# Expert 0's first slot tile taken from three batches, beside the routing of the last batch

## What is computed

```python
logits = np.einsum('bsd,de->bse', x, w_gate)
local_gate = 1.0 / (1.0 + np.exp(-np.einsum('bsd,de->bse', x, w_local).squeeze(-1)))
for b in range(B):
    prev_e = -1
    for s in range(S):
        fresh_e = int(np.argmax(logits[b, s]))
        e = fresh_e if s == 0 or local_gate[b, s] < 0.5 else (prev_e if prev_e >= 0 else fresh_e)
        prev_e = e
        h = np.maximum(x[b, s] @ w1[e], 0.0)
        out[b, s] = p[e] * (h @ w2[e])      # p is the softmax of logits[b, s]
```

## Time and profile before

| | |
|---|---|
| median of 3 runs | 882.67 us (881.75 to 883.35) |
| profiled execution | 882.88 us |
| its span, first to last instruction | 881.0 us |
| PE busy | 806.8 us, 92% of the span |
| POOL, DVE, ACT busy | 521.6, 447.2, 387.8 us |
| mean DMA rate | 140 GB/s |

### The profile page before, as it was taken

The page is one execution under the profiler, slowest core; times in us unless marked ns, Lnnn a source line. Parts: engine busy times, 40 slices in busy tenths (PEclk is TensorE's granted clock), DMA queues, the critical chain, the costliest instruction groups (busy, mean ns, idle before and its releaser), DMA issues. The chain is left out here.

```text
span 881.0 us, 16450 instructions
## 1 busy us (share of the span) xinstructions
PE 806.8 (92%) x5056; PEld 680.1 (77%) x5057; DVE 447.2 (51%) x1042; ACT 387.8 (44%) x667; POOL 521.6 (59%) x461
## 2 busy tenths in 40 slices
PE   6989999999999525999999999998488999999998
PEld 3768788788887314888888888886377899898998
DVE  5768888888878371222212221222085756645622
ACT  2658787887878331121212212121275534524310
POOL 4547767766778806845898989996265703404100
PEclk9999999999999956999999999999699999999999
DMA  7976787787674336574665655560310110110101
GB/s 184 343 181 172 188 197 181 175 199 192 166 169 120 114 128 215 160 256 167 239 181 187 179 190 166 192 227 36 114 36 19 48 61 25 38 47 1 47 10 54
DMA packets 78758, 123.42 MB, mean 140 GB/s; under 512 B 26176, under 2 KB 39744, under 8 KB 78720
## 3 DMA queue, kind: packets, MB, share of 16 engines
q1 hardware_dynamic: 68912, 100.13, 39.6%
q0 software_dynamic: 3472, 11.28, 4.3%
q10 hardware_dynamic: 6336, 11.54, 4.0%
HBM read 70.55 MB, written 23.86 MB: 107 GB/s over the span
## 5 line engine op out<-in xcount | busy, mean ns | idle before, releaser
L330 POOL TENSOR_SCALAR p_ring<-p_ring,xs_nat 128x576 f32<-128x576 f32 x144 | 105.9, 751 | 82.8 <-DVE xs_nat L437 82.8
L407 DVE TENSOR_REDUCE xs_nat<-psum 128x1 f32<-128x576 f32 x144 | 105.9, 749 | 44.4 <-PE psum L518 35.9
L422 DVE SCALAR_TENSOR_TENSOR p_ring<-psum,xs_nat,e_ring 128x576 f32<-128x576 f32 x144 | 114.5, 811 | 14.7 <-PE psum L564 9.6
L1166 PE MATMUL psum<-w_split,h_hi 128*128 x352 | 116.8, 403 | 3.2 <-DVE h_lo L1230 3.2
L518 PE MATMUL psum<-k_st,q_st 128*128 128x288 f32 x600 | 115.2, 318 | 4.5 <-issue 4.3
L1145 PE MATMUL psum<-w_split,x_hi 128*128 x352 | 117.3, 405 | 1.9 <-DVE x_lo L1225 1.9
L1072 POOL TENSOR_TENSOR w_split<-w_raw,w_split 128x1024 fp32r<-128x1024 f32 x48 | 115.4, 2404 | 4.0
L648 ACT ACTIVATE e_ring<-psum,xs_nat 128x576 f32<-128x576 f32 x144 | 105.7, 750 | 14.9 <-DVE xs_nat L407 14.0
L666 ACT COPY p_t<-psum 128x512 f32<-128x512 f32 x144 | 84.5, 587 | 32.4 <-PE psum L553 29.4
L518 PEld LDWEIGHTS psum<-k_st,q_st 128*128 128x128 f32 x600 | 85.5, 192 | 15.4 <-DVE p_ring L422 10.7
L1352 POOL TENSOR_TENSOR stage<-g,xs_nat 128x512 f32<-128x512 f32 (+1 forms) x20 | 27.3, 1365 | 110.0 <-ACT xs_nat L1558 110.0
(11 more groups left out here) (184 smaller groups left out, 1581.1 us busy)
## 6 DMA issues: line engine op xcount, KB each, us to landing
w_raw<-w_dram SPq DMA_DIRECT2D x48, 512.0 KB, 3.4
k_st<-k_split SPq DMA_DIRECT2D x60, 320.0 KB, 5.4
q_st<-q_split SPq DMA_DIRECT2D x60, 144.0 KB, 2.6
xs_dram<-stage SPq DMA_DIRECT2D x23, 256.0 KB, 2.3
xs_nat<-xs_dram ACTq DMA_DIRECT2D x22, 256.0 KB, 2.8
ys_dram<-y_nat ACTq DMA_DIRECT2D x22, 256.0 KB, 2.2
k_nat<-k_t_dram SPq DMA_DIRECT2D x15, 320.0 KB, 4.2
out_dram<-out_sb SPq DMA_DIRECT2D x32, 144.0 KB, 1.8
```

The source lines that it names most:

```text
L330: pl.tensor_scalar(t, t, rsum[:, col:col + 1], 1.0, ALU.mult, ALU.mult).then_inc(s_norm, 1)
L407: dve.tensor_reduce(negmax[:, u % 3, 0:1], s_bank[u % 3][:, :, 0:HALF], AX.XY, ALU.max, negate=True).then_inc(s_max, 1)
L422: dve.scalar_tensor_tensor(out=p_tile[u].rearrange("p (a b) -> p a b", a=2), in0=s_bank[u % 3][:, :, 0:HALF], scalar=thresh[:, u % 3:u % 3 ...
L1166: mm = pe.matmul(py, a[:, f, :], rhs.rearrange("p o n -> p (o n)"), start=(n == 0), stop=(n == len(terms) - 1))
```

## The change

- The three blocks up to the experts become one, with no barrier in between (`joined`). Everything `route` and `experts` need in SBUF is laid beside or over the attention's buffers (`place`).
- The routing is written anew in two halves, `last=0` for batches 0 to 2 and `last=1` for batch 3. Its pieces are called from the other engines' programs: DVE's `logits_early` and `fresh(0)` stand in pair 14, `rows(0)` in pair 15, and `early` behind the attention; PE's `rows`, `experts`, `ranks` and `first` for batches 0 to 2 stand in pair 15.
- `early` ends in the source rows of expert 0's first tile (`keep["ahead"][:, 0]`). POOL fetches that tile (`x_first`) before batch 3 is routed, and the hops of batch 3's routing stand between the matmuls of `up(0)` and `down(0)`. Tile 1's rows come from `next_tile`, all the others from `sources`.
- Expert 0's eight weight pieces are split one each in pairs 8 to 13 and two in pair 14; before one each in pairs 12 and 13, two in pair 14, three in pair 15 and one in the routing.
- Expert 1's low parts go from POOL to DVE (`low`), behind the routing; ACT's casts (`high`) stand between its work on tile 0. POOL gathers the tiles from the fourth on (23 of them, as before) in one run.
- There is one slot more (26 for 25), one zero-filled piece of 256 KB more, a second constant array of 128 KB (`order_const`), and a first one that is 125 columns wide for 339.

```diff
-SLOTS = (BATCH * SEQ - EXPERTS) // P + EXPERTS
+SLOTS = (BATCH * SEQ + P - EXPERTS) // P + EXPERTS
...
-        pair(ITER - 2, 0, pieces=((1, 0),))
-        pair(ITER - 2, 1, pieces=((1, 1),))
-        pair(ITER - 1, 0, pieces=((0, 2), (1, 3)))
-        pair(ITER - 1, 1, ahead=False, pieces=((0, 4), (1, 5), (1, 6)))
+        for r in range(6):
+            pair(ITER - 4 + r // 2, r % 2, pieces=((1, r),))
+        pair(ITER - 1, 0, pieces=((0, 6), (1, 7)))
+        routing["pool"]["constants"](pl)
+        pair(ITER - 1, 1, ahead=False)
...
+                if isinstance(i, int) and 2 * i + m == PAIRS - 2:
+                    routing["vector"]["logits"](dve)
+                if isinstance(i, int) and 2 * i + m == PAIRS - 1:
+                    routing["vector"]["rows"](dve, 0)
...
+    def early(v):
+        link(v, v.memset(e_row[0:EARLY, SEQ:ST * P], 0.0))
+        follow(v, 0)
+        for a in others:
+            link(v, v.memset(a[:], 1.0))
+            link(v, v.memset(a[:, :, 0:1], 0.0))
+        count(v, 0)
+        places(v, 0)
...
+        lanes(v, 0)
+        v.wait_ge(s_hop, 4)
+        token(v, keep["ahead"][:, 0:1], first_at, 1, "first")
...
+    def lanes(v, last):
+        at = columns(last)
+        for k in range(at.start, at.stop):
+            link(v, v.tensor_scalar(hot_lane[:, k, :], bf["lane"][:], lane[:, k:k + 1], None, ALU.is_equal), f"lane{k}")
...
+        transposes_x(0, x_first, s_first[0])
+        hop["rows"](pe, 1)
+        up(0, halves=range(1), part=range(0, 8))
+        hop["experts"](pe, 1)
+        up(0, halves=range(1), part=range(8, 12), ready=False)
+        hop["ranks"](pe, 1)
+        up(0, halves=range(1, 2), ready=False).then_inc(s_up, 1)
+        transposes_h(0)
+        hop["next"](pe)
+        down(0, part=range(0, 14))
+        hop["sources"](pe)
+        transposes_x(1, xs[:, 1, :], s_first[1])
+        down(0, part=range(14, 24), ready=False).then_inc(s_done, 1)
+        reached(pe, "tables")
+        up(1).then_inc(s_up, 1)
+        transposes_x(2, xs[:, 0, :], s_first[2])
         last = rounds(pe)
-        with pe.Fori(0, last) as j:
+        with pe.Fori(1, last) as j:
...
+        for r in range(3, 7):
+            high(r)
+        x_high(1)
+        high(7)
+        store(0)
+        relu(1)
+        x_high(2)
+        load(3)
...
+        h_low(0)
+        r["all_tiles"](v)
+        r["tables"](v)
+        x_low(1)
+        r["sources"](v)
+        r["weights"](v)
+        for n in range(4):
+            low(n)
+        y_out(0)
+        x_low(2)
+        for n in range(4, PIECES):
+            low(n)
```

More of the change, by code:

```diff
@@ L606, in pair @@
                 scores(n_i, n_m, 1)
+            if isinstance(i, int) and 2 * i + m == PAIRS - 1:
+                pe.wait_ge(s_mask, tile(i, m, 7) + 1)
+                routing["tensor"]["rows"](pe, 0)
             if here:
@@ L616, in pair @@
                 turned(i, m, 5)
+                if isinstance(i, int) and 2 * i + m == PAIRS - 1:
+                    routing["tensor"]["experts"](pe, 0)
                 values(i, m, 0)
@@ L631, in pair @@
                 turned(i, m, 8)
+                if isinstance(i, int) and 2 * i + m == PAIRS - 1:
+                    routing["tensor"]["first"](pe)
         pe.wait_ge(s_zero, 5)
@@ new lines, in route, with sources, weights @@
+    units_row = place("units_row", [1, SLOTS + 1], F32)
+    def sources(v):
+        v.wait_ge(s_hop, 9)
+        token(v, keep["source"][:], source_at, SLOTS, "source")
+    def weights(v):
+        link(v, v.scalar_tensor_tensor(out=tile[:], in0=tile[:], scalar=float(P), in1=lane[:], op0=ALU.mult, op1=ALU.add))
+        link(v, v.tensor_scalar(keep["index"][:].rearrange("p t b -> p b t"), tile[:].rearrange("p (b t) -> p b t", t=ST),
+                                -1.0, None, ALU.add))
+        v.wait_ge(s_exp, 1)
+        link(v, v.tensor_reduce(total[:], less, AX.X, ALU.add))
+        link(v, v.tensor_scalar(total[:], total[:], 1e-9, None, ALU.add))
+        link(v, v.reciprocal(total[:], total[:]))
+        for last in range(2):
+            at = columns(last)
+            link(v, v.tensor_tensor(sel[:, :, at], less[:, at, :].rearrange("p k e -> p e k"), hot[last][:], ALU.mult))
+        link(v, v.tensor_reduce(chosen[:], sel[:].rearrange("p e k -> p k e"), AX.X, ALU.add))
+        link(v, v.tensor_tensor(keep["weight"][:], chosen[:], total[:], ALU.mult), "weights")
@@ new lines, in reached @@
+    def reached(engine, name):
+        engine.wait_ge(step, STEP[name])
+    return {
+        "vector": {"logits": logits_early, "fresh": fresh, "rows": rows, "early": early, "last_logits": last_logits,
+                   "below_top": below_top, "follow": follow, "count": count, "places": places, "lanes": lanes,
+                   "tile_numbers": tile_numbers, "next_tile": next_tile, "next_source": next_source,
+                   "all_tiles": all_tiles, "tables": tables, "sources": sources, "weights": weights},
+        "tensor": {"rows": rows_pe, "experts": experts_pe, "ranks": ranks_pe, "first": first_pe, "next": next_pe,
+                   "sources": sources_pe},
+        "pool": {"constants": constants},
+        "scalar": {"exps": exps},
+        "reached": reached,
+    }
@@ L1722, in build @@
[L1722 to L1731 removed]
+                offset = [behind]
```

711 lines of the change are left out of this document (410 added, 301 removed).

## The result

| | median us | runs | ratio to before, 95% interval |
|---|---|---|---|
| before | 883.01 | 4 (881.75 to 883.74) | |
| after | 873.23 | 4 (872.13 to 875.36) | 0.9894 [0.9869, 0.9918] |
| forecast | 864.0 | range 858.5 to 872 | |

Faster, as forecast, but by 9.8 us instead of 18.8, and 1.2 us outside the range. The profiled execution after took 874.16 us with a span of 872.4. The changed kernel was measured in two more sessions and gave 873.30 and 872.54; the kernel before gave 888.92 and 881.11 beside it (0.9801 [0.9777, 0.9826] and 0.9902 [0.9873, 0.9931]). So the changed kernel repeats within 1 us, while the kernel before moves by several from session to session, and the gain came out at 9.8, 15.6 and 8.6 us.

A forecast was written before the change was run, and what follows sets the result against it. PE bounds attention and experts, with a routing hole near 310 us. Attention would end 2.6 + 1.9 us later, yet `down(1)` 18.8 us earlier (369.51 to 350.7), with nothing lost afterwards: 882.88 - 18.8 = 864.1; range 858.5 to 872.

The forecast's parts named there:

- behind the marker I cost everything at nothing: After the start of `down(1)`, no further loss: PE busy without a gap, weight splits ahead of need; 0 us.
- the marker: Start of `down(1)` on PE, up to which gain was summed; forecast to move from 369.51 to 350.7, 18.8 us less.
- The weight pieces: Attention: five pairs (8 to 12) with a POOL piece slowed by 0.43 each, 1.7 us later (0.4 to 2.6).
- The start: PE's wait for stacked keys near 48 us grows by 0.8 us from 0.28 MB more DMA (0 to 1.0).
- DVE in pairs 14 and 15: Seven more DVE instructions, about 2.7 us, mostly covered by its waits for PE; cost 0.1 us (0 to 1.5).
- The lanes and the order: Attention's end: last values wait for `first` and 15 lanes of 0.25 us; 1.9 us later (1.1 to 3.4).
- From the attention's end to the marker: Chain from 306.1: `up(0)` at 309.3, PE waits 336 to 340.1, low-clock `up(2)`, `down(1)` at 350.7.
- The gather chain as a rival: 23 gathered-tile stores delay POOL's splits for expert 7; 4.4 us free, decides from 3.3 us landing; chance 0.07.
- The rivals on the clock: PE's clock stays up after the attention: 861.8 us, or 858.8 if also through the later wait; chance 0.22.
- the clock stays up: Rival: `up(0)` at full clock ends 2.3 us earlier; without the second low stretch, 3.0 more; chance 0.22.
- the three signs of being wrong: PE waits at an expert's first tile, lanes take 0.35 or more, or a store lands in over 2.5 us.

The follow-up runs named there:

- e6: Changed kernel with expert 0's eight weight pieces loaded and split at pairs 12 to 15, as in the kernel before; 878.59 us.
- e10: Changed kernel with the copy of the first tile's result ahead of the weight pieces and three wide lane instructions; 871.40 us, 0.9780 of before.
- e7: The kernel before once more, unaltered, for a second trace of its first 60 us; 889.4 us, a single run.
- e5: Changed kernel with the 15 lane instructions of the first three batches made into three of five columns each; 870.90 us.
- e3: Changed kernel with the 15 small matmuls of the first tile's tokens issued behind the last values matmuls on TensorE; 876.85 us.
- e4: Changed kernel with VectorE's copy of the first tile's result ahead of the four weight pieces; 870.30 us, 0.9865 of before.
- e1: Changed kernel with 32 bytes more in front of all its SBUF buffers; 873.79 us, 0.9912 of before.
- e2: Kernel before with 32 bytes more, putting its operands where the changed kernel has them; 886.05 us, 1.0044 of before.
- e18: Changed kernel with the split weights 32 bytes lower and the operands where they are; 874.94 us.
- e9: Changed kernel unaltered, measured in the third session; 873.30 us, 0.9801 of before.
- e15: Changed kernel unaltered, measured in the fourth session; 872.54 us, 0.9902 of before.
- e11: e10 with 32 bytes more in front of all buffers; 871.22 us, 0.9778 of before.

## Why the prediction was right in sign and wrong in size

The step that failed is "behind the marker I cost everything at nothing"; 4.9 us are lost there. The other 5.3 are terms ahead of the marker that were mis-sized. Term by term:

*The weight pieces, 1.7 us (0.4 to 2.6).* Mis-sized, and outside the bounds: 3 to 4 us (A, e6). Pairs 8 to 11 do step by 17.2 as said, which gives the 1.7; pair 12 then takes 18.1 where 17.2 was forecast too. In this trace POOL's split of the keys comes late there (`k_st` 0.95 us late at 256.5). That a delay adds up in this way is read from the trace and was not tested by itself; e10 takes as long (17.95) without such a wait.

*The start, 0.8.* No cost shown and none excluded (e7). The profiled execution of before was a short one; the two profiled executions differ by 1.4 us at the group near 62 (60.13 and 61.53), and the comparison of the traces counts that against the change.

*DVE in pairs 14 and 15, 0.1.* From the group near 275 to the next it takes 8.66 to 8.68 before, 8.66 to 9.37 in the unshifted kernels with the pieces moved up: up to 0.7 (0.6 in the first trace), inside its bounds.

*The lanes and the order, values 1.9 later.* The lanes were 0.287, not 0.25, and not the 0.19 of the estimate beside it either. With the hops ahead of them the values stand 3.7 behind forecast, of which 2.5 come from the three terms above and 1.2 from here. Another 1.7 is the low clock under the values, a matter of the run (e5 and e3 have 1.95).

*From the attention's end to the marker.* The chain was right link by link: the wait for the copy and its store (4.1 forecast, 3.46 measured), the low `up(2)` behind it, the fetch within 0.4 of being needed. It was handed 5.2 us of lateness at `up(0)` (314.45 for 309.3) and passed 5.3 on at the marker: `up(0)` at the full clock gave 2.4 back, and the rest of the stretch to 340.90 took as much again, with `down(0)` starting at the low clock (0.76 for its first matmul) behind an idle time of 1.82. DVE's subtractions then begin at 337.88 for 332.7. e4 confirms the wait.

*Behind the marker everything at nothing.* This step failed. Its cover was that PE is busy without a gap, and PE was; but the matmuls themselves became slower. A tile is 0.18 us longer, 3.4 us by the last, by an address that no row of before could show; e1, e2 and e18 settle it. Another 1.8 us lies in the mixing. Of this some 0.9 is the same address, by the estimate above. The rest stays open: the mixing's length from its first transposes varies from trace to trace, 247.8 to 249.0 us in the three of the kernel before (e2 among them), 248.4 to 250.4 in the other seventeen.

*The gather chain as a rival.* It was put at 0.07, deciding only from 3.3 us a store, with 4.4 us of room. The stores took 2.76 us each instead of 2.63, 63.56 in all, and the room was nearly used up in two of three traces (e9, e15). With 18.8 us gained, expert 7's `up` would start at 554.3 (573.1 before), and in no trace without the early loads is its fourth piece split before 558.5. e10 and e11 show that case. So the forecast sum was out of this kernel's reach, as far as these traces tell; it took the copy, the wide lanes, the 32 bytes and the early loads, and then 864.4 us. That this is the forecast's 864 is luck, since that sum has neither the floor nor the address.

*The rivals on the clock* did not decide. The first half of "the clock stays up" came true in the profiled execution, where `up(0)` ran at the full clock (6.6 us, not 8.6), and not in e15, where it started low (0.76); the two executions took 874.16 and 873.49.

*The signs.* Of the three signs of being wrong, no wait at an expert's first tile and no lane of 0.35 were seen in the changed kernel; the stores' landing, with its bound of 2.5 us, had a median of 2.51 in the first trace and 2.35 in e15, so it told nothing.

## What to carry to other kernels

When a change moves a whole stage forward, work out for every later stage when its second engine can be done at the earliest (here GpSimd's splits, tied to the last of 23 stores), since that caps the gain and makes mends that are real one by one look worthless together. Profile the kernel before more than once: its start alone moved by 2.4 us, more than any term of the attention's side of the sum. When two kernels are compared, keep the two operands of each matmul at the same distance modulo 64 bytes, or a term enters that the diff's logic doesn't show.

## What the runs showed of the hardware

- Matmuls of 128x512 with a fresh 128x128 load each take 228 to 229 ns a step when the loaded operand and the streamed weights lie equal modulo 64 bytes, and 233 when they lie 32 bytes apart (12.28 to 12.33 us a tile against 12.49 to 12.52, in every trace of both kernels and their variants, waits left aside). Matmuls of 128x288 in the mixing take 134.0 and 134.7 ns a step.
- A DVE instruction of 0.18 us took 2.23 beside a POOL subtraction of 2.37 us, ending with it (e6).
- A PE wait of 4.55 us made its tile 7.3 us longer (e11), one of 2.08 us 3.9 (e10), as the matmuls behind it start at the low clock.
- PE stopped twice for about 1 us inside a row of ready matmuls in one trace (e7), while ACT and DVE stood too; not explained.
